# Up products of six expert steps by seven block products in place of eight, and down products taken piece by piece over four banks

## The reference

```python
scores = scale * q @ k.T                              # 4 batches, 8 heads, 576 x 576, head size 64
scores = where(scores >= rowmax(scores) - tau, scores, -1e9)
attn = softmax(scores)                                # divided by (row sum + 1e-9)
x = (attn @ v) as [2304 tokens, 512]
p = domain_probs / (domain_probs.sum(-1) + 1e-9)      # [2304, 4]
out = sum over 4 experts e of  p[:, e] * (relu(x @ w1[e]) @ w2[e])    # w1 512 x 1024, w2 1024 x 512
```

## Time and profile before

| what | value |
|---|---|
| median of 3 runs | 1091.63 us (1090.91 to 1091.88) |
| the profiled execution, its own time | 1088.7 us |
| its span, first to last instruction | 1086.7 us |
| granted TensorE clock | 1.0 (of full speed) |
| PE / DVE / ACT / POOL busy | 98 / 62 / 52 / 58% of the span |

### The profile page before, as it was taken

The page is one execution under the profiler, slowest core; times in us unless marked ns, Lnnn a source line. Parts: engine busy times, 40 slices in busy tenths (PEclk is TensorE's granted clock), DMA queues, the critical chain, the costliest instruction groups (busy, mean ns, idle before and its releaser), DMA issues.

```text
span 1086.7 us, 17018 instructions
## 1 busy us (share of the span) xinstructions
PE 1061.0 (98%) x5752; PEld 931.5 (86%) x5752; DVE 674.6 (62%) x1505; ACT 562.2 (52%) x990; POOL 629.0 (58%) x659
## 2 busy tenths in 40 slices
PE   5899999999999999999999999999999999999998
PEld 5789899899888888888899999988888888888887
DVE  6988788787887788777777878752122133343331
ACT  6776566666766647566475656644233232242330
...
GB/s 163 155 111 123 87 123 133 131 128 156 148 148 120 137 57 121 92 85 115 103 124 111 127 115 116 90 100 123 94 110 88 72 123 136 87 107 97 107 58 39
DMA packets 96788, 121.08 MB, mean 111 GB/s; under 512 B 41152, under 2 KB 45248, under 8 KB 96704
## 3 DMA queue, kind: packets, MB, share of 16 engines
...
q10 hardware_dynamic: 304, 0.33, 0.1%
...
## 4 chain that ended last, share of the span: by engine, by line
PE 92%; DVE 4%; issue 1%; ACT 1%; POOL 1%; DMA 1%; SPq 0%; ACTq 0%; DVEq 0%
PE e_ps L863 12%; PE e_ps L865 12%; PE e_ps L864 12%; PE e_ps L848 12%; PE e_ps L850 12%; PE e_ps L849 12%; PE t_ps L794 6%; PE s_ps L782 3%; PE x_ps L821 3%; PE s_ps L783 3%; PE x_ps L823 3%; PE x_ps L806 1%; DVE p L1002 1%; DVE small L991 1%; DVE q_hl L972 0%
## 5 line engine op out<-in xcount | busy, mean ns | idle before, releaser
L760 POOL TENSOR_TENSOR w_lo<-stage,w_hi 128x512 fp32r<-128x512 f32 x272 | 355.8, 1319 | 275.6 <-ACT w_hi L950 275.3
L950 ACT ACTIVATE w_hi<-stage 128x512 fp32r<-128x512 f32 x320 | 194.1, 625 | 177.3 <-PE e_ps L865 120.6
L848 PE MATMUL e_ps<-x_hi,w_hi 128*128 128x512 f32 (+1 forms) x640 | 241.3, 377 | 0.2 <-DVE h_lo L1042 0.2
L850 PE MATMUL e_ps<-x_hi,w_lo 128*128 128x512 f32 (+1 forms) x640 | 236.2, 369 | 0.0
L849 PE MATMUL e_ps<-x_lo,w_hi 128*128 128x512 f32 (+1 forms) x640 | 235.8, 368 | 0.0
L863 PE MATMUL e_ps<-w_hi,h_hi 128*128 128x512 f32 x576 | 229.8, 399 | 0.0
L865 PE MATMUL e_ps<-w_hi,h_lo 128*128 128x512 f32 x576 | 225.2, 391 | 0.0
L864 PE MATMUL e_ps<-w_lo,h_hi 128*128 128x512 f32 x576 | 224.8, 390 | 0.0
L1042 DVE SCALAR_TENSOR_TENSOR h_lo<-e_ps,h_hi 128x512 fp32r<-128x512 f32 (+1 forms) x160 | 101.8, 636 | 127.1 <-ACT h_hi L940 125.1
L940 ACT ACTIVATE h_hi<-e_ps 128x512 fp32r<-128x512 f32 (+1 forms) x160 | 88.6, 554 | 118.0 <-PE e_ps L850 117.2
L904 ACT ACTIVATE p<-s_ps,small 128x576 f32<-128x576 f32 x132 | 97.4, 738 | 73.2 <-DVE small L991 72.7
...
## 6 DMA issues: line engine op xcount, KB each, us to landing
stage<-w SPq DMA_DIRECT2D x320, 256.0 KB, 2.9
...
out<-acc SPq DMA_DIRECT2D x18, 256.0 KB, 2.0
...
v_raw<-v SPq DMA_DIRECT2D x80, 16.0 KB, 2.1
...
```

The source lines that it names most:

```text
L760: gp.tensor_tensor(w_lo[:, m % RING, :], stage[:, m % STAGES, :], w_hi[:, m % RING, :], ALU.subtract).then_inc(s_wl, 1)
L848: mm(ps[:, 0:n], w_hi[:, piece, tile], x_hi[:, k, cols], start=k == 0, stop=False)
L850: op = mm(ps[:, 0:n], w_lo[:, piece, tile], x_hi[:, k, cols], start=False, stop=k == KT - 1)
L950: run(w_hi[:, m % RING, :], stage[:, m % STAGES, :], copy).then_inc(s_wh, 1)
```

## The change

In steps 13, 14, 15, 17, 18 and 19 (`FAST`: the last two chunks but the first expert of each) the eight up groups become four "squares". A square is two up groups, that is 256 rows of h, by 512 tokens, by a contraction of 512. It is cut in halves three ways: 2 row groups, 2 halves of the contraction (256 each) and 2 halves of the tokens (256 each). The eight block products of that cut become seven, by the Strassen-Winograd scheme.

- **Products** (`m`): 7 of 6 matmuls each, 128x256, in place of 24 matmuls of 128x512. They go round all eight PSUM banks.
- **Sums of weights** (`a_load`, `a_sum`, `a_hi`, `a_lo`): the two raw up pieces of a square are loaded a second time by SP (2 DMAs of 256 KB), POOL makes four sums of 128x256, ACT the high part (128x1024), DVE the low part (128x1024, two inputs in SBUF).
- **Sums of tokens** (`t_sum`, `t_hi`, `t_lo`): once per chunk, nine POOL operations of 128x512, four copies on ACT, four subtractions on DVE.
- **Sums of products** (`keep`, `sum`): ACT copies the first product to SBUF; seven DVE additions of 128x256, each of a product in PSUM and a tile in SBUF, give the two row groups of h in SBUF.
- **h**: the top row's high part by ACT and low part by DVE (now with two inputs in SBUF); the lower row's high part by two ACT operations, its low part by POOL.
- **Low parts of weights** in the six steps: every odd piece by DVE, the rest by POOL.
- **Down products** in steps 12 to 19 (`WIDE`): four groups at once on four banks, in the order part 0 of groups 0 to 3, part 1 of groups 0 to 3 and so on, a part being two weight pieces; the ring places come free two by two (`s_w2`). The count of matmuls is the same.

The diff, cut to its core (leading blanks shortened):

```diff
+FAST = tuple(t for t in range((len(CHUNKS) - 2) * E, len(CHUNKS) * E) if t % E)
+WIDE = range(FAST[0] - 1, len(CHUNKS) * E)
+ROUND = (E - 1) * FT // 2
+QUAD = 256
...
 def lo_on_dve(m):
+    if m // PIECES in FAST:
+        return m % 2 == 1
     return m % 4 == 2 if m < E * PIECES else m >= DVE_FROM and m % 2 == 0
...
-    for m, g in enumerate(groups):
-        g.bank = m % 2
-        g.before = groups[m - 2] if m >= 2 else None
+    count, owner = 0, {}
+    for g in groups:
+        if g.kind == "down" and g.t in WIDE:
+            g.bank = g.j
+        elif g.t in WIDE and g.t not in FAST:
+            g.bank = 4 + g.j % 2
+        elif g.t not in WIDE:
+            g.bank = count % 2
+            count += 1
+        else:
+            continue
+        g.before = owner.get(g.bank) if g.bank < 4 or g.j >= 2 else None
+        owner[g.bank] = g
...
+ORDER_M = (1, 2, 6, 7, 5, 3, 4)
+MADE = {(sq.index, j): 5 * sq.index + count + 1 for sq in SQUARES for count, j in enumerate((1, 6, 7, 5, 3))}
...
+SUMMED = {2: 1, 6: 2, 7: 3, 5: 5, 3: 6, 4: 7}
+BANKS = 8
...
+        todo += [(mm(6, QUAD), "m", sq, j) for sq in SQUARES if sq.t == g.t for j in ORDER_M]
...
+            elif g.t in WIDE:
+    if g.j == 0:
+        todo += [(mm(6, D), "down", h, part) for part in range(4) for h in DOWN_GROUPS if h.t == g.t]
...
+        t_raw = [a[:, 0:512].rearrange("p (k n) -> p k n", n=QUAD) for a in (q_raw, k_raw, p[0], p[1], x_sum)]
+        t_hi = [a[:, 0:512].rearrange("p (k n) -> p k n", n=QUAD) for a in k_hh + q_hl]
+        t_lo = ([a[:, 0:512].rearrange("p (k n) -> p k n", n=QUAD) for a in k_ll]
+    + [a[:, 0:4, :].rearrange("p (k j) n -> p k (j n)", j=2) for a in v_hl])
+        m1 = x_sum[:, 0:QUAD]
+        u2, u3, u4 = (keep[:, i, :] for i in range(3))
+        c_top, c_low = (q_raw[:, 0:512], k_raw[:, 0:512]), (p[0][:, 0:512], p[1][:, 0:512])
+        banks = [s_ps[:, 0, :], s_ps[:, 1, :], x_ps[:, 0, :], x_ps[:, 1, :], e_ps[:, 0, :], e_ps[:, 1, :],
+     t_ps[:, 0:512], t_ps[:, 512:1024]]
...
+        def place(sq, j):
+            return banks[spot_of(sq, j) % BANKS][:, 0:QUAD]
...
+    elif name == "a_load":
+        sq, = x
+        if sq.index:
+            sp.wait_ge(s_a_sum, 4 * sq.index)
+        else:
+            sp.wait_ge(s_pv, len(PARTS))
+        for row in range(2):
+            sp.dma_start(a_raw[:, row * 512:(row + 1) * 512], w1[sq.t % E, 2 * sq.i + row]
+                         ).then_inc(s_a_ld, 16)
...
+    elif name == "t_sum":
+        r, i = x
+        t1, t2, t3, t4, b12 = t_raw
...
+        if i:
+            pool.wait_ge(s_t_sum, 9 * r + i)
+        elif r:
+            pool.wait_ge(s_hl_top, r * ROUND)
+            pool.wait_ge(s_hl_low, r * ROUND)
+        else:
...
+        out_, in0, in1, sign = (
+            (b12, tokens(x_hi, r, 0, 1).bitcast(F32), tokens(x_lo, r, 0, 1).bitcast(F32), ALU.add),
+            (t1, b12, b11_hi, ALU.subtract), (t1, t1, b11_lo, ALU.subtract),
+            (t3, b22_hi, b12, ALU.subtract), (t3, t3, b22_lo, ALU.add),
+            (t2, b22_hi, t1, ALU.subtract), (t2, t2, b22_lo, ALU.add),
+            (t4, b21_hi, t2, ALU.subtract), (t4, t4, b21_lo, ALU.add))[i]
+        gp.tensor_tensor(out_, in0, in1, sign).then_inc(s_t_sum, 1)
+    elif name == "a_sum":
+        sq, i = x
+        a11, a12, a21, a22 = (quarter(a_raw, k) for k in range(4))
+        s1, s2, s3, s4 = (quarter(a_sum, k) for k in range(4))
+        if i == 0:
+            pool.wait_ge(s_a_ld, 32 * (sq.index + 1))
+            if sq.index:
+                pool.wait_ge(s_a_lo, sq.index)
+            gp.tensor_tensor(s1, a21, a22, ALU.add).then_inc(s_a_sum, 1)
+        elif i == 1:
+            gp.tensor_tensor(s3, a11, a21, ALU.subtract).then_inc(s_a_sum, 1)
+        elif i == 2:
+            pool.wait_ge(s_a_sum, 4 * sq.index + 1)
+            gp.tensor_tensor(s2, s1, a11, ALU.subtract).then_inc(s_a_sum, 1)
+        else:
+            pool.wait_ge(s_a_sum, 4 * sq.index + 3)
+            gp.tensor_tensor(s4, a12, s2, ALU.subtract).then_inc(s_a_sum, 1)
+    elif name == "hlo_low":
+        sq, = x
+        row = 2 * sq.i + 1
+        pool.wait_ge(s_hh, sq.row1.index + 1)
+        gp.tensor_tensor(h_lo[:, row, :], c_low[sq.index % 2], h_hi[:, row, :], ALU.subtract
+                         ).then_inc(s_hl_low, 1)
...
+    elif name == "m":
+        sq, j = x
+        n = sq.index
+        first, second = sq.piece % RING, (sq.piece + 1) % RING
+        if j in (1, 4):
+            gp_lo, ve_lo = lo_counts(sq.piece + (j == 4))
+            pe.wait_ge(s_wl, gp_lo)
+            pe.wait_ge(s_wv, ve_lo)
+        room = occupant(sq, j)
+        if room and room[1] == 1:
+            pe.wait_ge(s_keep, room[0].index + 1)
+        elif not room and spot_of(sq, j) >= 4:
+            pe.wait_ge(s_acc, down_of(sq.t - 1, spot_of(sq, j) - 4).index + 1)
+        elif room:
+            pe.wait_ge(s_sum, 7 * room[0].index + SUMMED[room[1]])
...
+        if j == 6:
+            pe.wait_ge(s_a_lo, n + 1)
...
+        ps = place(sq, j)
+        left = {1: (w_hi[:, first, 0:QUAD], w_lo[:, first, 0:QUAD]),
+                2: (w_hi[:, first, QUAD:512], w_lo[:, first, QUAD:512]),
+                4: (w_hi[:, second, QUAD:512], w_lo[:, second, QUAD:512])}
+        for k, i in ((5, 0), (6, 1), (7, 2), (3, 3)):
+            left[k] = quarter(a_hi[:, n % 2, :], i), quarter(a_lo[:, n % 2, :], i)
+        right = {1: (tokens(x_hi, sq.round, 0, 0), tokens(x_lo, sq.round, 0, 0)), 2: (tokens(x_hi, sq.round, 1, 0), tokens(x_lo, sq.round, 1, 0)),
+                 3: (tokens(x_hi, sq.round, 1, 1), tokens(x_lo, sq.round, 1, 1)), 4: (t_hi[3], t_lo[3]),
+                 5: (t_hi[0], t_lo[0]), 6: (t_hi[1], t_lo[1]), 7: (t_hi[2], t_lo[2])}
+        (a_high, a_low), (b_high, b_low) = left[j], right[j]
+        for k in range(2):
+            tile = slice(k * P, (k + 1) * P)
+            mm(ps, a_high[:, tile], b_high[:, k, :], start=k == 0, stop=False)
+            mm(ps, a_high[:, tile], b_low[:, k, :], start=False, stop=False)
+            op = mm(ps, a_low[:, tile], b_high[:, k, :], start=False, stop=k == 1)
+        op.then_inc(s_up if j in (2, 4) else s_m, 1)
...
+    elif name == "a_hi":
+        sq, = x
+        act.wait_ge(s_a_sum, 4 * sq.index + 4)
+        if sq.index >= 2:
+            act.wait_ge(s_m, MADE[sq.index - 2, 3])
+        run(a_hi[:, sq.index % 2, :], a_sum[:], copy).then_inc(s_a_hi, 1)
+    elif name == "keep":
+        sq, = x
+        act.wait_ge(s_m, MADE[sq.index, 1])
+        if sq.index:
+            act.wait_ge(s_sum, 7 * sq.index - 5)
+        run(m1, place(sq, 1), copy).then_inc(s_keep, 1)
+    elif name == "hhi_top":
+        sq, = x
+        act.wait_ge(s_sum, 7 * sq.index + 6)
+        run(h_hi[:, 2 * sq.i, :], c_top[sq.index % 2], ACT.Relu).then_inc(s_hh, 1)
+    elif name == "hhi_low":
+        sq, = x
+        act.wait_ge(s_sum, 7 * sq.index + 7)
+        run(c_low[sq.index % 2], c_low[sq.index % 2], ACT.Relu).then_inc(s_relu, 1)
+        act.wait_ge(s_relu, sq.index + 1)
+        run(h_hi[:, 2 * sq.i + 1, :], c_low[sq.index % 2], copy).then_inc(s_hh, 1)
...
+            elif t in WIDE and i < PIECES - 2:
+                act.wait_ge(s_w2, 3 * (t - WIDE[0]) + (i - FT) // 2 + 1)
...
+    elif name == "a_lo":
+        sq, = x
+        dve.wait_ge(s_a_hi, sq.index + 1)
+        ve.tensor_tensor(a_lo[:, sq.index % 2, :], a_sum[:], a_hi[:, sq.index % 2, :], ALU.subtract
+                         ).then_inc(s_a_lo, 1)
+    elif name == "sum":
+        sq, i = x
+        n = sq.index
+        top, lower = c_top[n % 2], c_low[n % 2]
+        if i == 0:
+            if n >= 2:
+                dve.wait_ge(s_hl_top, n - 1)
...
+            dve.wait_ge(s_up, sq.row0.index + 1)
+            dve.wait_ge(s_keep, n + 1)
+            add = quarter(top, 0), place(sq, 2), m1
+        elif i == 1:
+            dve.wait_ge(s_m, MADE[n, 6])
+            if n:
+                dve.wait_ge(s_sum, 7 * n)
+            add = u2, place(sq, 6), m1
+        elif i == 2:
...
+            add = u3, place(sq, 7), u2
+        elif i == 3:
...
+            add = u4, place(sq, 5), u2
+        elif i == 4:
+            if n >= 2:
...
+            add = quarter(lower, 1), place(sq, 5), u3
+        elif i == 5:
...
+            add = quarter(top, 1), place(sq, 3), u4
+        else:
...
+            add = quarter(lower, 0), place(sq, 4), u3
+        out_, in0, in1 = add
+        ve.tensor_tensor(out_, in0, in1, ALU.add).then_inc(s_sum, 1)
+    elif name == "hlo_top":
+        sq, = x
+        dve.wait_ge(s_hh, sq.row0.index + 1)
+        ve.scalar_tensor_tensor(out=h_lo[:, 2 * sq.i, :], in0=c_top[sq.index % 2], scalar=0.0,
+                                in1=h_hi[:, 2 * sq.i, :], op0=ALU.max, op1=ALU.subtract
+                                ).then_inc(s_hl_top, 1)
```

(40 more changed lines are left out.)

220 lines of the change are left out of this document (202 added, 18 removed).

## The result

The change made the kernel slower: 1097.38 us (median of 20 runs, 1091.89 to 1102.15) against 1091.18 us (20 runs, 1088.51 to 1092.39) before, a ratio of 1.0057 with the interval 1.0047 to 1.0066. The forecast was 1083.8 us, in a range of 1081 to 1093.

A forecast was written before the change was run, and what follows sets the result against it. PE's own stream was taken as the bound: 1088.7 - 9.6 (stream) + 1.5 (DVE peaks) + 0.3 (end) = 1080.9 us profiled, 2.9 us under the median, so 1083.8 us; range 1081 to 1093.

The forecast's parts named there:

- PE's stream: Up products: 42 matmuls at 0.120 us replace 24 at 0.2268 in each of 24 squares, -9.6 us.
- The rival with 0.112 us: Long runs of narrow matmuls reach at the lowest the 192-wide pace, time 1073.8 us; chance 0.02.
- a pace of 0.189 us set by the weight loads: Rival: PE's weight loads set the products' pace, +60 us, 1151; chance 0.02.
- The downs and the end: Down order costs nothing by itself; closer last stores may overlap partly, +0.3 us.
- 24.3 us of work: DVE's count during four squares taking PE 20.2 us; lag and downs give room, allowance +1.5 us.
- over 90%: Sign to look for: DVE busy more than this share while squares run.
- an overhang of 2 us goes under the downs: POOL has 22 us of work in the squares' 20.2; the excess was expected to be hidden.
- covered by pieces 14 places ahead: SP's 48 more loads, with weight loads queued behind waits for `a_sum`, were priced at 0.
- weights come late: One of the signs that would show the forecast wrong; no size given.
- `t_sum` in step 12 or 16 at 0: POOL's token sums, 11.6 us per chunk, have one step to themselves and cost nothing.
- The slower rival: Loop through DVE and ACT makes squares 7.25 us, 25 us in all, 1107.5 us; chance 0.11.
- the gain is partly eaten: Rival: DVE's SBUF pairs cost 0.7 to 2.5 us a step, time 1088.3, range 1086 to 1097; chance 0.20.

The follow-up runs named there:

- e5: Changed kernel with seven eighths of each POOL `a_sum` operation left out from the second square on; 1081.38 us, ratio 0.9908 to the kernel before.
- e9: Changed kernel with DVE's `a_lo`, `hlo_top` and weight low parts cut to 32 columns in the fast steps; 1081.81 us, ratio 0.9917 to the kernel before.
- e7: Changed kernel with all up products as before the change, keeping only the piecewise downs on four banks; 1091.50 us, ratio 1.0000 to the kernel before.
- e1: Changed kernel with each square's second raw weight load issued from ACT's queue in place of SP's; 1091.32 us, ratio 1.0001 to the kernel before.
- e3: Changed kernel without the second raw weight loads for all squares but the first; 1085.39 us, ratio 0.9949 to the kernel before.
- e2: Changed kernel with the nine token sums per chunk on DVE in place of POOL, same places in the order; 1092.07 us, ratio 1.0005.
- e8: Changed kernel with measured planner durations, token sums made and planned on DVE, and second loads issued by ACT; 1094.11 us, ratio 1.0028 to the kernel before.
- e10: Changed kernel with measured planner durations and token sums made and planned on DVE, second loads on SP; 1094.29 us, ratio 1.0023 to the kernel before.
- e11: Changed kernel with the planner letting POOL's operations and DVE's SBUF pairs take turns in the last two chunks; 1094.00 us, ratio 1.0020.
- e4: Changed kernel with the planner's durations set to those in the trace, changing only queue orders; 1086.10 us, ratio 0.9959 to the kernel before.

## Why the prediction was wrong, point by point

**PE's stream: right.** 0.120 us a matmul, 20.19 us for four squares, -9.6 us; e5 has -9.85 and e9 -9.7 when nothing is late. The rival with 0.112 us is refuted, and so is a pace of 0.189 us set by the weight loads. They are listed as busy for 20.18 of the 20.19 us of the squares, but overlap one another; whether they have a share in the 0.120 no run shows. The gap formula of the Trainium skill ("TensorE: Matmul & The Clock Gate", "Back-to-back issue gap"), 109 ns at 256 columns, doesn't give the pace here: 168 matmuls in a row lay 0.120 us apart. The section itself offers it for an isolated matmul, and gives about 131 ns at 512 columns for a stream with weight loads, where this case has 227.

**The downs and the end: right at 0**, and 0 in place of the +0.3 for the stores (e7).

**DVE: a pair's price right, its load counted too high, and not the first suspect.** I had 24.3 us of work in the squares' 20.2. DVE was busy 17.64 of 20.19 us in step 13 and 17.32 of 23.01 in step 14, that is 87 and 75%, where "over 90%" was to be seen. The pairs came out: 0.69 + 0.42 us against 1.06 on average for pairs of 512, and 1.32 for `a_lo`. The sums did not: 22 of them and not 28 began in the squares, and in a row they start 0.33 us apart and not 0.43:

```profile
829.57 0.41 DVE L1488 TENSOR_TENSOR p<-e_ps,keep 128x256 f32<-128x256 f32 x1
829.90 0.41 DVE L1488 TENSOR_TENSOR q_raw<-e_ps,keep 128x256 f32<-128x256 f32 x1
```

DVE held PE by its order, where a waiting `a_lo` or `w_lo` stood ahead of a sum. It also has a part in the chain below: in step 18 the third square's `a_hi` was done at 1007.8, but its `a_lo`, for which the last square's `a_sum` waited, began at 1009.57, behind accumulations, a low part of 1.55 us and seven sums.

**POOL: here the forecast failed.** The step was "its weights are ring places ahead and `a_sum` is due 11 us before its use, so an overhang of 2 us goes under the downs". Being due early doesn't let it start early. There is one `a_sum` tile, so a square's sums wait for the `a_lo` of the square before, and that `a_lo` waits for an `a_hi` tile which a product of two squares before must release. For the third and fourth square this chain runs inside the up part: the sixth product of the first square, which frees the third's `a_hi` tile, is done at 828.3, `a_lo` of the fourth at 841.3, needed at 840.6. In it are four sums of 1.06 to 1.19 us, not 0.68, mainly because the price that POOL pays to DVE's pairs was taken into POOL's total and not into the length of the chain. The 0.68 is also a slip: its own working, 1.29 less 256 columns at 2.2 ns, gives 0.73, which is what a sum takes when nothing disturbs it. POOL was busy only 15.5 of 23 us in step 14: a load count could not show it.

**SP's queue: priced at 0, wrong.** "0, covered by pieces 14 places ahead": the ring is 14 places ahead, but the loads are issued just in time behind `a_load`, and I didn't follow who stands behind ACT's `whi` and DVE's `w_lo` when their piece is late: `keep` and the sums, and so PE. The prediction's own sign, "weights come late", shows: ACT waited 71.5 us for them from 780 us on, against 26.0 before. Freed of it (e1) the kernel won 6 us, and 12 with the loads gone altogether (e3).

**`t_sum` in step 12 or 16 at 0: wrong in step 16**, where the stalls are 5.1 us and e2 took 4.0 of them away, right in step 12 (39.3 us of POOL in 43.5, no stall).

**The clock: not in the sum.** Two falls cost 3.3 of the 14.8 us.

**The rivals.** The slower rival had the right kind (queues of ACT and DVE that hold each other and PE, `keep` among what is held) but the wrong start: not DVE's sums and `hhi_low`, but POOL's sums, by way of `a_hi`, `a_lo` and `whi`. Its chance of 0.11 was too low; the count of single tiles would have raised it. The rival "the gain is partly eaten" had DVE falling behind as its cause; DVE's pairs cost what the mean said, and their harm went through POOL.

**Open.** How much of the late `a_sum` is conflict and how much single tiles. No run has a second `a_sum` tile: the tiles of the fast steps fill the space of the attention's tiles exactly, without room for 4 KB more a partition. Why e8 and e10 are worse than their parts, and e11 than e4, is not known beyond where their stalls stand. Stalls are read from one profiled execution of each kernel, and differ between executions; the medians are the firmer numbers.
